# Decay tables made on the chip's VectorE as running products, in a three-stage f32 kernel on one core

## The reference, cut to what matters

```python
# q, k, v: (2, 8, 768, 64); lam: (8,), between 0.97 and 0.99
for b in range(nb):                       # blocks of positions, one after the other
    qb, kb, vb = (q[:, :, sl], k[:, :, sl], v[:, :, sl])
    intra = einsum('bhic,bhjc->bhij', qb, kb) * where(rel >= 0, lam ** rel, 0)
    inter = einsum('bhid,bhde->bhie', qb * lam ** (pos + 1), kv_state)
    out[:, :, sl] = einsum('bhij,bhjd->bhid', intra, vb) + inter
    kb_dec = kb * lam ** (block - 1 - pos)
    kv_state = lam ** block * kv_state + einsum('bhsd,bhse->bhde', kb_dec, vb)
# then  u = x + real(fft2(x)), LayerNorm, relu(un @ w_ch1) @ w_ch2, and  (sigmoid(conv) * (x @ w_val)) @ w_out
```

## Time and profile before

| | us |
|---|---|
| median of 3 runs | 440.9 |
| the runs | 440.57, 440.9, 441.8 |
| the profiled execution, its own time | 442.06 |
| its span in the trace | 440.3 |
| PE busy, of the span | 433.4 |
| DVE, ACT, POOL busy | 252.5, 152.9, 145.9 |

### The profile page before, as it was taken

One profiled execution on the slowest core, in us unless ns is written; L12 is line 12 of the kernel. 1 busy time (PEld: TensorE's weight loads), 2 busy tenths in 40 slices (PEclk: granted clock), 3 DMA queues, 4 the chain that ended last, 5 costly groups with the idle time before them and its releaser, 6 DMA issues.

```text
span 440.3 us, 7188 instructions
## 1 busy us (share of the span) xinstructions
PE 433.4 (98%) x2940; PEld 415.6 (94%) x2940; DVE 252.5 (57%) x433; ACT 152.9 (35%) x289; POOL 145.9 (33%) x99
## 2 busy tenths in 40 slices
PE   8999989999999999999999999999999999999997
PEld 8888879899999999999999999999999999989986
DVE  1545999855338835354423327948557548889220
ACT  1145442472231411113442335362233251616222
POOL 1344442359234223322646332243224272000000
DMA  5988720232113020202203302202102110001212
GB/s 182 307 260 292 244 74 1 96 97 98 49 46 97 22 75 25 72 21 76 98 0 97 95 1 95 82 15 97 69 28 95 45 52 1 1 1 71 73 48 95
DMA packets 13504, 36.27 MB, mean 82 GB/s; under 512 B 1552, under 2 KB 2840, under 8 KB 13472
## 3 DMA queue, kind: packets, MB, share of 16 engines
q1 hardware_dynamic: 13456, 35.81, 24.4%
q10 hardware_dynamic: 16, 0.02, 0.0%
HBM read 32.66 MB, written 3.15 MB: 81 GB/s over the span
## 4 chain that ended last, share of the span: by engine, by line
PE 90%; DVE 6%; DMA 2%; issue 1%; ACT 0%; SPq 0%; DVEq 0%
PE ps L559 10%; PE ps L561 10%; PE ps L582 10%; PE ps L581 10%; PE ps L580 10%; PE ps L560 10%; PE ps L660 3%; PE ps L662 3%; PE ps L661 3%; PE ps L682 3%; PE ps L684 3%; PE ps L683 3%; PE ps L429 2%; PE ps L467 1%; DMA chunks<-in_qkv 1%; PE ps L513 1%
## 5 line engine op out<-in xcount | busy, mean ns | idle before, releaser
L772 ACT ACTIVATE hh<-ps 128x384 fp32r<-128x384 f32 x64 | 31.5, 495 | 170.7 <-PE ps L561 170.7
L1044 DVE SCALAR_TENSOR_TENSOR hl<-ps,hh 128x384 fp32r<-128x384 f32 x64 | 35.3, 556 | 90.5 <-ACT hh L772 90.5
L559 PE MATMUL ps<-cen_h,w1h_a 128*128 128x384 f32 x128 | 43.8, 342 | 0.0
L559 PE MATMUL ps<-cen_h,w1h_b 128*128 128x384 f32 x128 | 43.6, 341 | 0.0
L561 PE MATMUL ps<-cen_h,w1l_b 128*128 128x384 f32 x128 | 43.2, 337 | 0.0
L582 PE MATMUL ps<-hh,w2l_b 128*128 128x384 f32 x128 | 43.1, 337 | 0.0
L581 PE MATMUL ps<-hl,w2h_b 128*128 128x384 f32 x128 | 43.1, 337 | 0.0
L580 PE MATMUL ps<-hh,w2h_b 128*128 128x384 f32 x128 | 43.1, 337 | 0.0
L560 PE MATMUL ps<-cen_l,w1h_a 128*128 128x384 f32 x128 | 43.1, 337 | 0.0
L561 PE MATMUL ps<-cen_h,w1l_a 128*128 128x384 f32 x128 | 43.1, 337 | 0.0
L560 PE MATMUL ps<-cen_l,w1h_b 128*128 128x384 f32 x128 | 43.0, 336 | 0.0
(11 more groups left out here) (169 smaller groups left out, 1011.8 us busy)
## 6 DMA issues: line engine op xcount, KB each, us to landing
raw_a<-in_mlp SPq DMA_DIRECT2D x16, 512.0 KB, 4.7
raw_b<-in_mlp SPq DMA_DIRECT2D x16, 512.0 KB, 4.4
chunks<-in_qkv SPq DMA_DIRECT2D x12, 512.0 KB, 5.9
chunks<-in_qkv SPq DMA_DIRECT2D x22, 256.0 KB, 5.6
out<-out_sb SPq DMA_DIRECT2D x11, 256.0 KB, 2.0
raw_a<-in_val SPq DMA_DIRECT2D x2, 512.0 KB, 4.3
raw_b<-in_out SPq DMA_DIRECT2D x2, 512.0 KB, 4.4
seq_c<-const_seq SPq DMA_DIRECT2D x1, 768.0 KB, 7.5
```

The lines of the kernel that those rows point to most:

```text
L559: mm(bank, wh_, xh, start=r == 0, stop=False)
L772: nc.scalar.activation(hh[:, slot, j], ps[j][:, 0:TB], ACT.Relu).then_inc(s_hh, 1)
L1044: stt(hl[:, slot, j], ps[j][:, 0:TB], 0.0, hh[:, slot, j].bitcast(F32), ALU.max, ALU.subtract).then_inc(s_hl, 1)
```

## The change

The table is no longer carried by DMA. lam is loaded to every partition (`lam_all`, [128, 8]; `lam_mine` picks the four of a partition's half). POOL makes an identity matrix of ones by `affine_select`. DVE then makes each head's table [128, 128] with one running product along the row, out[t] = out[t - 1] * lam + identity[t] (`tensor_tensor_scan`, 8 of them), and after `mask(0)` the query powers by four more, out[t] = out[t - 1] * lam + 0, from 1. The HBM tensor, `heads`, `spread_powers` and the copy of ACT are gone. The tables run in the other direction, so the indices of their readers turn round. SP issues the loads of the first three chunks without a wait, with the values of chunk 0 ahead of the keys and queries of chunk 1. On PE `scores(0)` follows the first 8 warm products, 2 more stand behind it, and `scores(1)` comes after `from_chunk(0)`, in the common banks and behind `mask(0)`; `scores(2)` follows directly and waits for both halves of `mask(1)`. `chunk_pair(0, 1)` stands one turn earlier on DVE.

```diff
@@ program
-    WARM_KEYS = 4
-    WARM_TABLE = 8
+    WARM_KEYS = 2
-    rv_dram = nc.dram_tensor("powers_dram", (H, 2 * P), F32, kind="Internal").ap()
+        identity = esum[:, 0]
+        lam_all, lam_mine = esum[:, 1, 0:H], esum[:, 1, H:H + HP]
@@ sync
-            sp.dma_start(rv[:, P - 1:P], lam.rearrange("(h a) -> h a", a=1)).then_inc(s_lam, 16)
+            sp.dma_start(lam_all, bass.AP(tensor=lam.tensor, offset=0, ap=[[0, P], [1, H]])).then_inc(s_lam, 16)
             load(0, 0, 2, s_tin)
-            sp.wait_ge(s_pow, 2 + 7)
-            sp.dma_start(rv_dram, rv).then_inc(s_rv, 16)
             load(0, 2, 3, s_kin)
-            sp.wait_ge(s_rv, 16)
-            sp.dma_start(decay[:, :, :],
-                         bass.AP(tensor=rv_dram.tensor, offset=1, ap=[[1, P], [2 * P, H], [1, P]])).then_inc(s_tab, 16)
+            load(0, 3, 4, s_vin)
             load(1, 0, 2, s_tin)
-            load(0, 3, 4, s_vin)
             load(1, 2, 3, s_kin)
             load(2, 0, 2, s_tin)
@@ tensor, scores
-                if n >= 2:
-                    pe.wait_ge(s_pr, 2 * n if n > 2 else 2)
+                if n >= 1:
+                    pe.wait_ge(s_pr, 2 * n)
@@ tensor
             keep_warm(WARM)
-            spread_powers()
+            scores(0)
             keep_warm(WARM_KEYS)
-            scores(0)
-            scores(1)
-            keep_warm(WARM_TABLE)
             for n in range(N):
                 if n == 0:
                     state_product(0)
-                if 1 <= n < N - 1:
+                    from_chunk(0)
+                if n + 1 < N:
                     scores(n + 1)
@@ scalar
-            act.dma_start(heads, head_tab).then_inc(s_heads, 16)
-            act.wait_ge(s_spread, 1)
-            copy(qpow, ps[SPEC][:, 0:HP * P].rearrange("p (a n) -> p a n", a=HP)).then_inc(s_qpow, 1)
@@ vector
-            for e in range(7):
-                w = 1 << e
-                tt(rv[:, P - 2 * w:P - w], rv[:, P - w:P], rv[:, P - w:P - w + 1].broadcast_to([H, w]),
-                   ALU.mult).then_inc(s_pow, 1)
+            for par in range(2):
+                rows = slice(par * Dh, (par + 1) * Dh)
+                nc.vector.tensor_copy(lam_mine[rows], lam_all[rows, par::2]).then_inc(s_mine, 1)
+            scan = nc.vector.tensor_tensor_scan
+            dve.wait_ge(s_eye, 1)
+            for par in range(2):
+                for h in range(par, H, 2):
+                    scan(decay[:, h], lam_all[:, h:h + 1].broadcast_to([P, P]), identity, 0.0,
+                         ALU.mult, ALU.add).then_inc(s_tab, 1)
             mask(0)
+            zero = u_pad[0][:, 0, 0:1].broadcast_to([P, P])
+            for hp in range(HP):
+                scan(qpow[:, hp], lam_mine[:, hp:hp + 1].broadcast_to([P, P]), zero, 1.0,
+                     ALU.mult, ALU.add).then_inc(s_qpow, 1)
@@ vector, loop
                 if n == NC - 1:
                     chunk_pair(0, 0)
+                    chunk_pair(0, 1)
                 if n == NC:
-                    chunk_pair(0, 1)
                     two_even(0)
@@ gpsimd
+            nc.gpsimd.memset(identity, 1.0).then_inc(s_one, 1)
+            pool.wait_ge(s_one, 1)
+            nc.gpsimd.affine_select(identity, identity, [[1, P]], ALU.is_equal, 0.0, base=0,
+                                    channel_multiplier=-1).then_inc(s_eye, 1)
-            pool.wait_ge(s_tab, 16)
+            pool.wait_ge(s_tab, H)
```

More of the change, by code:

```diff
@@ L53, in constants, with program @@
     seq_tab = np.concatenate(parts, 1).astype(np.float32)
-    half = np.arange(P) >= P // 2
-    head_tab = [np.arange(2 * H)[:, None] == 2 * a + half[None, :] for a in range(H)]
-    return seq_tab, hid_tab, np.concatenate(head_tab, 1).astype(np.float32)
-def program(nc, qkv, lam, w_mlp, w_val, conv_w, w_out, seq_tab, hid_tab, head_tab, out):
+    return seq_tab, hid_tab
+def program(nc, qkv, lam, w_mlp, w_val, conv_w, w_out, seq_tab, hid_tab, out):
     B, S, D = out.shape
@@ L583, in mlp_out @@
                     m.then_inc(s_ch, 1)
-            def spread_powers():
-                pe.wait_ge(s_heads, 16)
-                pe.wait_ge(s_pow, 2 + 7)
-                for hp in range(HP):
-                    cols = slice(hp * P, (hp + 1) * P)
-                    m = mm(ps[SPEC][:, cols], heads[:, cols], rv[:, 0:P], start=True, stop=True)
-                m.then_inc(s_spread, 1)
             pe.wait_ge(s_set, 1)
             keep_warm(WARM)
-            spread_powers()
+            scores(0)
             keep_warm(WARM_KEYS)
-            scores(0)
-            scores(1)
-            keep_warm(WARM_TABLE)
             for n in range(N):
@@ L611, in _ @@
                     hid_transform(n - 1)
-                from_chunk(n)
+                if n:
+                    from_chunk(n)
                 if n == N - 3:
```

43 lines of the change are left out of this document (19 added, 24 removed).

## The result

The changed kernel takes 435.12 us (median of 4 runs, 434.64 to 435.9) where the kernel before takes 441.21 (median of 4, 440.57 to 441.8). The ratio is 0.9864, 95% interval 0.9843 to 0.9885: faster by 1.4%, 6.1 us. The forecast was 433.6 with a range of 432.3 to 438.3.

What follows compares the result with a forecast made beforehand. PE, busy 433.4 of 440.3 us, was taken as the bound, with room mostly in the first 18 us. 6.9 from the start plus 0.4 from the moved pair gave 7.3, so 433.6 against the 440.9 median; range 432.3 to 438.3.

Steps and rivals of the forecast that it cites:

- The bound and the mark: PE bounds the kernel; the start of `scores(2)`, at 18.38 us before, moves the end by as much as it moves.
- The start: PE up to the third scores: `scores(2)` starts at 11.45 us against 18.38, 6.9 us earlier.
- The clock: PE during the first scores: clock rises from lower to upper level at about 6.4 us, between 5.1 and 7.9.
- the transfers: Load queue at the start: 340 to 381 GB/s, kr and vr of chunk 0 by 6.2 us, chunk 1 at 7.2.
- The running products: DVE at the start: eight at 0.35 us each, 2.8 together, table ready at 5.8 us (4.6 to 7.8).
- The new wait for the second mask: PE ahead of `scores(2)`: it waits for `mask(1)` behind `scores(1)`, costing 1.3 us.
- The moved pair: `chunk_pair(0, 1)` in DVE's idle time: `radix4(5)` 0.54 us later, net 0.4 us earlier (0.5 lost to 1.2 gained).
- The sum and the median: Whole kernel: 6.9 + 0.4 = 7.3 us; profiled 442.06 lies 1.2 over the median, so 433.6 against 440.9.
- rival 1: PE's start: clock stays low through the chain, only 1.8 us gained there, 438.7 us; chance 0.14.
- rival 3: Start loads late: at 200 GB/s chunk 1 arrives at 10.5 us instead of 7.2, 435.1 us; chance 0.08.
- The dear running products: Rival on DVE: one every 0.60 us, table at 7.85, 5.3 us gained, 435.2 us; chance 0.10.
- the slower end: Rival: twelve running products ahead of `mask(1)` delay `scores(2)`; gain gone at 1.09 us each, 443.4 at 1.3; chance 0.04.

Runs made afterwards that it cites:

- experiment 7: Changed kernel with the eight running products of the table made twice: 438.99 us (10 runs), ratio 0.9959 to the kernel before.
- experiment 8: Kernel before with SP's loads issued without waits and ScalarE issuing the table's write and read-back, table still by DMA: 445.43 us, ratio 1.0092.
- experiment 1: Changed kernel with `chunk_pair(0, 1)` put back in its old turn: 435.97 us, ratio 0.9903 to the kernel before.
- experiment 11: Changed kernel run again, nothing altered: 434.72 us (6 runs), ratio 0.9873 to the kernel before.
- experiment 9: Changed kernel with the second scores in banks of their own and placed between `state_product(0)` and `from_chunk(0)`: 434.3 us, ratio 0.985 to the kernel before.
- experiment 10: Changed kernel with own banks for the second scores and `scores(1)` ahead of `state_product(0)`, the old order on PE: 434.99 us, ratio 0.9877 to the kernel before.
- experiment 3: Changed kernel with the second scores in two banks of their own, third scores waiting for the first mask only: 434.58 us, ratio 0.9865 to the kernel before.
- experiment 2: Kernel before with only `chunk_pair(0, 1)` moved one turn ahead: 439.83 us (9 runs), ratio 0.9978.
- experiment 12: Kernel before run again, nothing altered, for a second profile: median 441.13 us of 8 runs, profiled execution 442.98.
- experiment 5: Changed kernel without any warm products, neither the 8 nor the 2: 436.09 us, ratio 0.9877 to the kernel before.

## Why the prediction was right, and where it was off

*The bound and the mark:* right, as long as the clock is up at the third scores; the first table above shows it. Where it isn't (experiments 7 and 8), the mark is the fourth scores.

*The start, forecast 6.9, measured 6.14.* The difference of 0.79 us adds up so: 0.07 is that the forecast counted from the chain's 18.38 and not from the timeline's 18.31; `from_chunk(0)` started 0.5 late (8.55, not 8.05); it passed PE on to the second scores 0.08 later than allowed; and from the start of the second scores to the mark it is 2.64, not 2.50. That last piece is the second mask, which starts 0.04 us after the scores end, while the third scores start 0.15 after the mask ends, so that PE stood for 1.48 and not 1.3.

Behind these stand three terms. The first scores started at 5.41, not 4.77: chunk 0 landed later. Ahead of it is lam's DMA, now in 128 pieces, and right behind it are the next loads; which of the two holds it back was not taken apart. The clock was forecast to rise at 6.4, and had risen by 5.41 (in experiment 1 it had not by 7.6, so this term is a matter of the execution). And the keys came at 6.9, where I had them by 6.2: that made `state_product(0)` the step that `from_chunk(0)` waits for, not the mask. This too is in part a matter of the execution, since in the second profile of the changed kernel (experiment 11) the keys were there with the table, and the mark is at 11.81, 6.5 us ahead of 18.31.

Of these the term that failed by its reason is the transfers. I put them at 340 to 381 GB/s from 2.4 us on, and took the landing of the first load from a profile in which nothing was behind it. The queue moved 287, 262 and 207 GB/s in the windows from 3 to 6 us and 375 only from 6 to 7. The same error is larger further on, where it hardly shows: chunk 1 was forecast for 7.2, and in experiments 9 and 10, where PE waits for it, the second scores start only at 9.49 and 9.06. In the changed kernel `from_chunk(0)` ends at about that time, so the path felt none of it; that is luck. The 0.6 us that the working allows for a landing to be reported stands in no row, and no run took it apart.

*The running products, forecast 0.35 us each, measured 0.33.* Right: an operation of as many elements comes every 0.20 us, and the 0.13 more are one further step of 1.04 ns for each of the 128 elements. This agrees with the half throughput that the Trainium skill states for `tensor_tensor_scan` ("DVE: opcode table, instruction layouts, handler registers and perf-mode slots", section 6, Datapath and trigger behaviour).

*The new wait for the second mask:* right in place and price; experiment 3 shows that it is on the path, and that 0.8 to 0.9 of its 1.48 us can be had back.

*The moved pair, forecast 0.4, measured 0.83.* Right in kind, and the working had the start of the second pair, the later `radix4(5)` and PE's added wait as they came. What was mis-sized is the way back: I gave back the gain at `mask(8)`, which was to wait for the scores until 50.2 on the old scale. It did (0.34 us, and it starts at 44.12, 6.54 us before its old 50.66, so 0.40 more than the 6.14 of the start). The other 0.43 comes right behind it: the first operation of `two_odd` takes 1.04 us where it took 1.47 in the kernel before. The usual time is 0.69. It lies beside POOL's product of the queries for 0.5 us where it lay beside it for 0.9, and it is longer by 0.35 and by 0.78. The same is seen at the start of experiment 1, where one of the four running products of the query powers takes 1.21 us instead of 0.40 beside POOL's product of the keys; the masks, which read PSUM, keep their 0.6 each beside POOL. That POOL is the cause was read from the timelines and not tested. I had stopped the working at `mask(8)` and called the remainder unchanged.

*The sum and the median.* 7.3 was forecast from the profiled execution, and between the profiled executions 7.06 was measured: 0.24 off. Against the medians it is 6.1, and the forecast of the time missed by 1.5 us. The step that failed is "it lies 1.2 over the median, so against 440.9 it is 433.6": it took for granted that the profiled execution of the changed kernel would lie as far over its median. It lies 0.1 under it. The sum of marks puts such differences into the start: the kernel before has times from 439.1 to 443.5 over all comparisons here, the changed kernel from 434.6 to 436.4.

The granted clocks of the runs of the kernel before fit this. Those with a mean of 0.992 take 442.4 to 443.5 us. 0.992 is what 6.6 us at half the clock give in 440, as in experiments 2 and 12, where the clock was lost in a gap. Those with 0.999 or 1.0 fall into two heaps, 439.1 to 441.0 and 441.9 to 442.3, and the profiled execution (442.06, 0.999) belongs to the upper: a late mark for its kernel. But no execution of the old kernel faster than 441.77 has a trace, so where the others gain is inferred. Nor is it excluded that the profiler itself makes this kernel's start late: all four profiled executions with the table by DMA (before, 2, 8 and 12) lie 0.9 to 1.9 us over their medians, while those with the new table lie on both sides. The prediction left room for "the moment at which the clock rises" in the changed kernel and did not ask how the profile of before stood in this.

*The rivals.* The low clock (rival 1, forecast 438.7 if all of the chain stays at it) did not come in that form in any trace of the changed kernel. In experiment 1 the clock rose only in `from_chunk(0)`, and the time was 1.2 us longer; without any warm product the median is 0.85 to 1 us longer. Its mechanism is real, as experiment 7 shows, where the slow chain to 19 us goes with 3.8 us more. The transfers (rival 3) came in kind: where PE waited for chunk 1 it landed at 9.1 to 9.5, between the 7.2 of the forecast and the 10.5 of that rival, but in the changed kernel its reader was as late, and only the 0.5 us at `from_chunk(0)` was felt. The dear running products and the slower end did not happen; experiment 7 gives their slope: 2.7 us of added work cost 2.3 at the best and 6 at the worst, against the 2.6 that the prediction's formula has for eight products.

## What to carry to other kernels

A small table that is sent through HBM costs more than its bytes: it holds the queue that issues it, and when it was moved to another queue beside the large loads it came 7.5 us later still (experiment 8); make it on an engine that is idle at that time, and then let the loads go. Before a gain from a profile is taken off a median, find out where in its kernel's scatter the profiled execution lies: here one mark, the start of the fourth scores, gave the time of all fourteen profiled executions within 0.12 us. Where two groups of work wait for the same mask, ask first whether the second can have banks of its own.

## What the runs showed of the hardware that was not expected

- TensorE's clock at the start differs between executions of the same kernel, and the PEclk column does not show the slow stretch at the beginning: it is 1.00 in every window of the first 12 us of the profiles before and after, with groups of 2.08 and of 1.16 us in them. A clock that falls later it does show: 0.50 from 11 to 17 us in experiment 2. In the kernel before, 16 warm records from 13.5 to 14.0 us took 3.13 us in one execution and 3.78 in two; its first scores took 2.08 in one and 1.16 in two. Both of the early ones had lost the upper clock by the end of a gap of 3.8 and 4.2 us (PEclk 0.50 from 11 to 17 us in both).
- Work at the start that comes earlier and faster can cost time: those two executions have the later mark.
- The upper clock was reached without any warm product, by 4.6 us after the first matmul and with 0.3 us of idle time between (experiment 5), and was not reached until 19 us with eight of them where an idle 1.8 us followed (experiment 7).
- Between the issue of a DMA of 8 KB to HBM and that of the read that waits for it lie 1.3 us with the queues nearly empty (4.04 to 5.35), and 6.8 us with the loads of more than two chunks issued from another queue at the same time (experiment 8).
- Running products over 128 elements follow each other every 0.33 us on DVE, in f32, on 128 partitions; one that fell beside POOL's product of the keys took 1.21 us (experiment 1).
